# Attention with complex decay and two MLPs on one core: one activation table for logarithm and exponential, the decay chain two positions earlier, masks behind the next chunk's products in the first slots

## The reference, cut to what matters

```
mag = sqrt(a_re^2 + a_im^2);  scale = min(mag, 0.999) / (mag + 1e-6)
a = (a_re + i a_im) * scale
S = a[:, None] * S + outer(k, v);  y = q @ real(S)
h = x @ w_in;   g = h * clip(h + 3, 0, 6) / 6;      x2 = g @ w_out
h = x2 @ w2_in; g = max(h, 0) + alpha * min(h, 0);  out = g @ w2_out
```

## Time and profile before

| | us |
|---|---|
| median of 3 runs | 1179.44 (1177.57 to 1180.14) |
| the profiled execution, its own time | 1178.28 |
| its span | 1176.5 |
| TensorE busy | 1001.9 |
| VectorE busy | 638.5 |
| ScalarE busy | 590.5 |
| GpSimd busy | 307.0 |
| mean granted TensorE clock | 0.939 |

### The profile page before, as it was taken

The page is one execution under the profiler, slowest core; times in us unless marked ns, Lnnn a source line. Parts: engine busy times, 40 slices in busy tenths (PEclk is TensorE's granted clock), DMA queues, the critical chain, the costliest instruction groups (busy, mean ns, idle before and its releaser), DMA issues.

```text
span 1176.5 us, 17999 instructions
## 1 busy us (share of the span) xinstructions
PE 1001.9 (85%) x6882; PEld 973.2 (83%) x6882; DVE 638.5 (54%) x1116; ACT 590.5 (50%) x957; POOL 307.0 (26%) x291
## 2 busy tenths in 40 slices
PE   0247676898888889899898889999999999999998
PEld 0246575887887878888787889999999999999998
DVE  3755676666666666666576651455344343434432
ACT  6837666677677677676676733533121121212221
POOL 2213321111221211212222123333333333333332
PEclk9868888899999998988899999999999999999999
DMA  5350222222222222222222214210110101101000
GB/s 167 109 159 16 61 62 64 83 69 67 77 69 66 81 63 74 71 74 67 80 63 61 68 35 170 86 41 1 41 41 1 41 1 41 41 1 41 1 21 21
DMA packets 77862, 70.54 MB, mean 60 GB/s; under 512 B 32592, under 2 KB 73552, under 8 KB 77392
## 3 DMA queue, kind: packets, MB, share of 16 engines
q1 hardware_dynamic: 77776, 69.39, 20.6%
HBM read 40.90 MB, written 9.44 MB: 43 GB/s over the span
## 4 chain that ended last, share of the span: by engine, by line
PE 43%; DVE 21%; ACT 20%; issue 10%; SPq 3%; DMA 1%; DVEq 0%; ACTq 0%
PE op L1018 7%; PE op L1020 7%; PE op L1019 7%; PE hp L1018 7%; PE hp L1020 7%; PE hp L1019 7%; DVE gated L772 4%; DVE t_fb L722 3%; DVE t_phase L694 3%; ACT gate L551 2%; ACT L508 2%; ACT L499 2%; DVE prod L737 2%; ACT L514 2%; DVE scores L744 2%
## 5 line engine op out<-in xcount | busy, mean ns | idle before, releaser
L458 POOL TENSOR_TENSOR g_lo<-gated,g_hi 128x384 fp32r<-128x384 f32 x256 | 273.1, 1067 | 767.6 <-ACT g_hi L558 767.6
L558 ACT ACTIVATE g_hi<-gated 128x384 fp32r<-128x384 f32 x256 | 133.8, 523 | 411.4 <-DVE gated L786 290.6
L782 DVE TENSOR_SCALAR gate<-hp,alpha_sb 128x384 f32<-128x384 f32 x128 | 79.1, 618 | 229.6 <-PE hp L1020 229.6
L772 DVE SCALAR_TENSOR_TENSOR gated<-gate,hp 128x384 f32<-128x384 f32 x128 | 70.3, 550 | 183.3 <-ACT gate L551 183.2
L1018 PE MATMUL hp<-x_hi,wa_hi 128*128 128x384 f32 x384 | 135.3, 352 | 35.5 <-DVE gated L772 32.9
L1018 PE MATMUL op<-g_hi,wb_hi 128*128 128x384 f32 x384 | 144.0, 375 | 9.7 <-ACT out_sb L563 8.9
L985 PE MATMUL gp<-st 96*128 96x128 f32 x192 | 39.7, 372 | 121.0 <-DMA st<-prod 121.0
L985 PEld LDWEIGHTS gp<-st 96*128 96x128 f32 x192 | 34.5, 267 | 126.6 <-DMA st<-prod 126.6
L1019 PE MATMUL op<-g_lo,wb_hi 128*128 128x384 f32 x384 | 137.1, 357 | 0.0
L1020 PE MATMUL op<-g_hi,wb_lo 128*128 128x384 f32 x384 | 136.5, 355 | 0.0
L1020 PE MATMUL hp<-x_hi,wa_lo 128*128 128x384 f32 x384 | 131.3, 342 | 0.0
(11 more groups left out here) (101 smaller groups left out, 1947.9 us busy)
## 6 DMA issues: line engine op xcount, KB each, us to landing
st<-prod SPq DMA_DIRECT2D x96, 145.1 KB, 2.9
a_sb<-a_in SPq DMA_DIRECT2D x24, 288.0 KB, 3.4
qk_sb<-qk_in SPq DMA_DIRECT2D x24, 288.0 KB, 3.4
v_pad<-v_in SPq DMA_DIRECT2D x24, 192.0 KB, 3.0
x<-out_sb SPq DMA_DIRECT2D x8, 576.0 KB, 3.4
x_raw<-x SPq DMA_DIRECT2D x8, 576.0 KB, 4.7
out<-out_sb SPq DMA_DIRECT2D x8, 576.0 KB, 3.1
st<-prod SPq DMA_DIRECT2D x96, 32.2 KB, 2.2
```

Source lines behind the costliest of these rows:

```text
L458: pool.tensor_tensor(g_lo[:, at, :], gated[:, at * UT:(at + 1) * UT], g_hi[:, at, :].bitcast(F32), ALU.subtract).then_inc(glo_done, 1)
L558: act.activation(g_hi[:, at, :], gated[:, at * UT:(at + 1) * UT], ACT.Copy).then_inc(ghi_done, 1)
L772: dve.scalar_tensor_tensor(out=gated[:, to], in0=gate[:, at], scalar=1.0, in1=hp[:, n % 2, 0:UT], op0=ALU.min, op1=ALU.mult).then_inc(gate ...
L782: dve.tensor_scalar(gate[:, at], hp[:, n % 2, 0:UT], 0.0, alpha_sb[:, m:m + 1], ALU.min, ALU.mult).then_inc(gate_done, 1)
```

## The change

- `logs` first loads the table set `natural_log_exp_and_others`; `angle` still loads `trig_and_small`.
- ScalarE: `logs` and `copy_ends` go from position 2 to 1, `inverses` from 3 to 2, `squares` from 4 to 3, `angle` from position 0 of the next slot to 4, `waves` from position 1 to 0.
- VectorE: `mags` goes from position 0 of the next slot to 4. `residue`, `refine` and `ratio` stand together at position 3 (2 in slots up to 2), `lost` and `decays` at 4 (2 in slots up to 2).
- In slots up to 2 (`early`) the masks stand behind the products of the next chunk, and `x_high` behind `inverses`.
- For chunk 2 (`CPU - 1`) two of the twelve stack transfers are issued by ScalarE, the others by SP.

```diff
--- before.py
+++ after.py
@@ -103,6 +103,11 @@
         for pos in range(max(POSITIONS, len(items))):
             yield (s, pos, items[pos] if pos < len(items) else None, chunk_at(s), chunk_at(s + 1), chunk_at(s + 2),
                    chunk_at(s + 3))
+
+
+def early(s):
+
+    return s < CPU
 
 
 def is_first(c):
@@ -352,7 +357,7 @@
                 for to, rows in low_stack(c, 0) + high_stack(c, 0):
                     sp.dma_start(to, rows).then_inc(st_landed[c % 2], 16)
                 sp.wait_ge(prod_done, 2 * c + 2)
-                for to, rows in low_stack(c, 1) + high_stack(c, 1):
+                for to, rows in high_stack(c, 1) + ([] if c == CPU - 1 else low_stack(c, 1)):
                     sp.dma_start(to, rows).then_inc(st_landed[c % 2], 16)
 
             def store_x2(u):
@@ -494,6 +499,7 @@
                 act.activation(flat(t_abs, 0), flat(a_sb[:, c % 2, :, :, :], 1), ACT.Abs).then_inc(abs_set, 1)
 
             def logs(c):
+                act.preload_act_table_set("natural_log_exp_and_others")
                 act.wait_ge(m2_done, c + 1)
                 need(act, inv_done, c)
                 act.activation(t_log[:, :, :, :], t_sq[:, :, :, :], ACT.Ln).then_inc(log_set, 1)
@@ -534,6 +540,12 @@
                 act.activation(flat(t_trig, 0), flat(t_trig, 0), ACT.Sin, bias=half_pi[:, 0:1], scale=-TWO_PI
                                ).then_inc(trig_set, 1)
 
+            def stack(c):
+                act.wait_ge(ends_set, c + 1)
+                act.wait_ge(prod_done, 2 * c + 2)
+                for to, rows in low_stack(c, 1):
+                    act.dma_start(to, rows).then_inc(st_landed[c % 2], 16)
+
             def copy_k(c, k):
                 act.wait_ge(k_turned, 2 * kept(c) + k + 1)
                 need(act, kv_ready, kept(c))
@@ -588,27 +600,35 @@
                 keeps = c0 is not None and not is_last(c0)
                 if n is not None:
                     gate_of(n + GSTEP)
-                if pos == 0 and c1 is not None:
-                    angle(c1)
-                if pos == 1 and c1 is not None:
-                    waves(c1)
-                if pos == 2 and c0 is not None:
+                if pos == 2 and c0 is not None and not early(s):
                     x_high(c0)
                 if n is not None:
                     high(n + GSTEP)
-                if pos == 0 and keeps:
-                    copy_k(c0, 0)
-                if pos == 1 and keeps:
-                    copy_k(c0, 1)
-                if pos == 2:
+                if pos == 0:
+                    if keeps and not early(s):
+                        copy_k(c0, 0)
+                    if c1 is not None:
+                        waves(c1)
+                    if keeps and early(s):
+                        copy_k(c0, 0)
+                if pos == 1:
+                    if keeps:
+                        copy_k(c0, 1)
                     if c1 is not None:
                         copy_ends(c1)
+                        if c1 == CPU - 1:
+                            stack(c1)
                     if c2 is not None:
                         logs(c2)
-                if pos == 3 and c2 is not None:
-                    inverses(c2)
-                if pos == 4 and c3 is not None:
+                if pos == 2:
+                    if c2 is not None:
+                        inverses(c2)
+                    if c0 is not None and early(s):
+                        x_high(c0)
+                if pos == 3 and c3 is not None:
                     squares(c3)
+                if pos == 4 and c2 is not None:
+                    angle(c2)
                 for w in splits_at(s, pos):
                     split_w(w)
                 if n is not None and n % MT_FF == MT_FF - 1:
@@ -813,34 +833,38 @@
             for s, pos, n, c0, c1, c2, c3 in places():
                 if n is not None:
                     gate1(n + GSTEP)
+                if c0 == 0 and pos == 0:
+                    dve.wait_ge(masks_set, 4)
                 if pos == 0:
-                    if c2 is not None:
-                        mags(c2)
                     if c1 is not None:
                         phases(c1)
                         fractions(c1)
-                    if c0 is not None:
-                        if c0 == 0:
-                            dve.wait_ge(masks_set, 4)
+                    if c0 is not None and not early(s):
                         mask(c0, 0)
                         mask(c0, 1)
-                if pos == 1 and c1 is not None:
-                    if c1 == 0:
-                        dve.wait_ge(pads_set, 3)
-                    forward(c1)
-                    backward(c1)
-                    products(c1)
+                if pos == 1:
+                    if c1 is not None:
+                        if c1 == 0:
+                            dve.wait_ge(pads_set, 3)
+                        forward(c1)
+                        backward(c1)
+                        products(c1)
+                    if c0 is not None and early(s):
+                        mask(c0, 0)
+                        mask(c0, 1)
+                if pos == (2 if early(s) else 3) and c2 is not None:
+                    residue(c2)
+                    refine(c2)
+                    ratio(c2)
+                if pos == (2 if early(s) else 4) and c2 is not None:
+                    lost(c2)
+                    decays(c2)
                 if pos == 2 and c0 is not None:
                     x_low(c0)
                     if not is_last(c0):
                         state(c0)
-                if pos == 3 and c2 is not None:
-                    residue(c2)
-                if pos == 4 and c2 is not None:
-                    refine(c2)
-                    lost(c2)
-                    ratio(c2)
-                    decays(c2)
+                if pos == 4 and c3 is not None:
+                    mags(c3)
                 if s == CPU - 1 and pos == POSITIONS - 1:
                     for k in range(GSTEP):
                         gate1(k)
```

## The result

The changed kernel takes 1065.76 us (median of 4, 1064.19 to 1071.88) beside 1178.92 of the kernel before on the same chip: ratio 0.905, 95% interval 0.902 to 0.908. The forecast was 1068. The profiled execution is the slowest of the four: 1071.88, span 1070.2, clock 0.981. Both stand in the table, since profiles of one kernel differ by 2 to 3 us.

What follows compares the result with a forecast made beforehand. No single engine bounds; the order in which ScalarE and VectorE hand over work keeps TensorE above its floor. Savings 3.9 + 11.3 + 6.3 + 22.4 + 66.9 = 110.8 off 1178.3 give 1067.5, so 1068 us; range 1047 to 1098.

Steps and rivals of the forecast that it cites:

- Switch and loads: ScalarE table loads: five a chunk become two, 1.31 us a switch, 3.9 a chunk; first scores 3.9 earlier.
- Rival 3: The common table has no square, so a load returns ahead of the squares: about 1094 us; chance 0.05.
- Ring A: Steady slots, ScalarE and VectorE: from `gated` of position 1 to the next one, 22.4 us.
- Ring B: Steady slots, stack transfers: `gated` through product, issue, landing, scores and hidden matmuls to the gate, 21.1 to 22.9 us.
- Ring C: Steady slots, TensorE's own work: 22.7 us on average, 21.7 with 5 items and 24.8 with 6.
- Interlock: Three rings within a microsecond cause some waits and low clock: steady slots 24.0 us on average, fifteen intervals 360.
- Rival 1: Every slot keeps a wait over 2 us, the clock falls after it, slots stay 25.6: 1092 us; chance 0.20.
- Rival 2: TensorE becomes the bound, without waits and at full clock, 22.7 us a slot: 1044 us; chance 0.10.
- First interval of the first slots: From scores 0 to the next scores, bound by stack, q/k issue, landing, scaling and first product: 14.8 us.
- Second interval: The next interval, up to scores 2, running through ScalarE: 14.8 us; both intervals together 29.6 for 40.9.
- Masks, outputs and the state: First slots: these come some 6 us later against the products, claimed hidden behind the stack.
- Chunk 2 to the first hidden matmul: Scores 2 to first hidden matmul, 12.5 us for 9.1; the second part, to scores 3, 29.7 for 39.4.

Runs made afterwards that it cites:

- e7: The changed kernel with one more exponential on ScalarE, into a spare tile, ahead of every chunk's inverses: 1069.38 us, ratio 0.9063.
- e12: The changed kernel with the second half of the stack transferred in the old order, low parts first and high parts last: 1057.82 us, ratio 0.897.
- control: The changed kernel once more, unaltered, as the level for other runs: 1066.87 us, ratio 0.9054.
- e3: The changed kernel with `early` False for every slot, so the first slots have the steady order too: 1072.61 us, ratio 0.909.

## Why the prediction was right, and where it was not

The mechanism was right: three rings, ScalarE's blocked one opened by fewer loads and by logs and angle in idle time, both waits of TensorE reduced, and everything won before the last scores kept to the end (477.7 against 479.2). The time was right to 2 us of 1068, and that closely by luck: up to the scores of chunk 8 the two profiles took 11 to 13 us more than forecast, behind them 8 to 9 less.

- **Switch and loads.** 1.31 each, three less a chunk: first scores at 39.47 and 39.25 instead of 42.65, -3.2 to -3.4 for -3.9. Rival 3 (a load for the squares) did not happen.
- **Ring A, 22.4.** The stations stand within 0.1 of where they were put, in a slot of 22.57. The count was right, but by e7 this is the ring with room.
- **Ring B, "1.30 until the scores start".** Wrong: 2.07 in the slot shown, 2.08 in the median. The step failed at reading the diff; I took its line on the stack for one that concerns chunk 2 alone. It cost 9 us in all by e12, 2 of them by way of the clock in the fifteen intervals. The five intervals before chunk 8 are its clearest trace: 116 forecast, 121 measured, 116.45 in e12.
- **Ring C, 22.7.** TensorE is busy 22.7 an interval in after and 22.6 in e12. The other figure for its floor, 23.8, was read too high: it took the two longest waits (2.9 a slot) for all idle time. By the view of busy time by stretch TensorE idled 53.6 / 15 = 3.6 and was busy 24.9, at a clock of 0.92, which makes 22.9 at full clock.
- **Interlock, "23.2 with 5 items and 25.6 with 6".** The ten intervals of five items average 23.20, the five of six items 24.25. So the 6.8 us by which this term was too large are those of six items. In three of these (24.85, 24.83 and 24.85) TensorE does not idle at all and is alone the bound, 24.8 by my own count of ring C, and I had put 0.8 of interlock on top. The other two (23.66 and 23.06) belong to the last chunk of a batch, which keeps no state: 188 matmuls and not 212, a difference that the forecast did not make. That the 23.2 of five items was met is luck: with the landing that I had assumed (e12) they average 22.59, so this term was 0.6 too large as well, and the longer landing and one slot at the low clock filled it up. Announced were waits under 1.5 a slot and a clock over 0.95; both hold.
- **Rival 1** (after a wait of over 2 us the clock falls and stays low) happened in one slot of the fifteen, in the nineteenth slice of the page: scores 19 started after a wait of 1.97 for their stack, and by the view of busy time by stretch the clock was then 0.50 (the 1.2 GHz level) for 5 us, with 20 matmuls in them. The wait alone does not explain it. Scores 13 of the same execution started after a wait of 1.99 and the clock stayed at 1.00, with 36 matmuls in the same 5 us. First behind scores 19, then behind scores 13:

```profile
496.23:501.23 5.00, 5.00 (x20) 5.00 (x21) 4.30 (x9) 2.49 (x6) 1.00 (x1) 0.50 0.70 186
501.23:506.00 4.77, 4.77 (x29) 4.74 (x28) 1.07 (x2) 1.41 (x3) 0.00 (x0) 0.81 0.02 3
506.00:512.00 6.00, 6.00 (x97) 5.55 (x96) 5.66 (x12) 4.62 (x8) 1.14 (x1) 1.00 0.00 0
```
```profile
356.63:361.63 5.00, 5.00 (x36) 5.00 (x37) 4.35 (x10) 2.37 (x6) 1.01 (x1) 1.00 0.66 172
```

The interval behind scores 19 lasted 26.64; in e12 the same one is 22.63.
- **Rival 2** is nearly e12, with 23.1 a slot. What keeps it at 1058 and not at 1044 is spread evenly: its scores 3 come at 116.3 and not 110.5, chunks 3 to 8 take 116.45 and not 111, and the fifteen intervals 346.6 and not 340.5.
- **First interval of the first slots, 14.8.** 15.5, of which 0.4 goes in e12.
- **Second interval, 14.8.** 17.5 and 16.0. "Masks, outputs and the state ... hidden behind the stack they no longer hold" failed. The chain of waits of e12, in which the landing is short, shows what is late there:

```profile
62.02 1.21 DVE scores L764 x2
...
63.27 3.64 PE yp L1030 x64
66.92 2.74 PE gp L1037 x16
...
70.27 0.56 DVE s_pad L782
...
70.97 2.05 PE gp L1009 x8
```

Masks behind the products mean outputs and state (6.4 us on TensorE) and then VectorE's new state before the next scores, from 62.0 to 70.8, as long as the stack itself. In the profile of after the last landing, 4.21 us in place of 2.6, ended later still (72.47).

- **Chunk 2 to the first hidden matmul, 12.5.** 15.4. In the chain of after:

```profile
78.13 1.28 ACT L502
...
80.82 0.52 ACT wb_hi L580
...
81.78 1.33 DVE t_log L685
...
84.29 1.55 DVE t_eps L701
...
87.29 0.56 DVE x_lo L770
87.89 0.69 PE hp L1042
```

Logs to decays of chunk 3, 9.2 us with a weight split and two VectorE steps at 1.33 and 1.55, while GpSimd splits weights (both take 0.55 in a steady slot), stand ahead of `x_low`. That is the price of having them out of the way of the first gates; I had put 3.4 more for it (12.5 for 9.1), and it was 6.3. ScalarE then waits for the gates, 3.33 and 2.09:

```profile
91.18 0.58 ACT L563 ACTIVATE gate<-hp,half 128x384 f32<-128x384 f32 x1 [3.33 <-PE hp L1044]
93.85 0.58 ACT L563 ACTIVATE gate<-hp,half 128x384 f32<-128x384 f32 x1 [2.09 <-PE hp L1044]
```

The second half, 29.7, measured 30.5.

What stays open: why the clock fell behind scores 19 and not behind scores 13; why the runs of one kernel lie up to 8 us apart (1064.19 to 1071.88 in after, 1064.64 to 1070.39 in the control), where those of e3 lie within 1.7; and what the doubled transposes do before chunk 3.

## What to carry to other kernels

Split a stretch into busy time and idle time of the engine that should bound it, with its clock: here 44% of the gain in the steady slots was the same number of matmuls at a higher clock, a gain that no sum of removed waits contains. Do the same when two runs that differ by a small edit are compared, since one slot at the low clock can hold more of the difference than all the others (3.6 us of 6.1 in e12). Close each ring station by station and then ask which of them has slack by adding work to it; the one that I could time best was not the one that bound. Read every line of a diff for all its cases: the order of the last transfers of a group decided here when the group had landed, and the small one last was worth 9 us.

## What the runs showed of the hardware

The page of after (KB each, us from issue to landing) has the stack's pieces:

```profile
st<-prod SPq DMA_DIRECT2D x94, 145.1 KB, 2.9
...
st<-prod SPq DMA_DIRECT2D x96, 32.2 KB, 1.9
```

A group of twelve is as late as its last piece: 2.08 from the end of the last issue to the scores with 145 KB last (after), 1.32 with 32 KB last (e12). From the start of that last issue to its landing the medians of chunks 8 to 23 are 2.63 and 1.84. The Trainium skill ("DMA: Bandwidth & Descriptors", Anatomy of one DMA) gives a fixed 2.0 us and a further bytes / 436 KB per us for a transfer issued by GpSimd. By it the two sizes would differ by (145 - 32) / 436 = 0.26 us; an estimate from that page, made for another issuer than the one here. The rows for SP's queue show more: 1.0 between the medians of the page of after (0.7 in that of before, 2.9 and 2.2), and 0.75 in the ring.
